# Reciprocal sums of an attention tile turned narrow and early, and spread through DRAM

## What is computed

```python
scores = scale * np.matmul(q, k.transpose(0, 1, 3, 2))
scores = np.where(keep, scores, -1000000000.0)
scores = scores - np.max(scores, axis=-1, keepdims=True)
a = np.exp(scores)
a = a / (np.sum(a, axis=-1, keepdims=True) + 1e-09)
return np.matmul(a, v).astype(np.float32)
```

## Time and profile before

| | |
|---|---|
| median of 3 runs | 562.24 us (561.69 to 562.94) |
| the profiled execution, its own time | 562.56 us |
| its span, first to last instruction | 560.8 us |
| granted TensorE clock, mean | 0.997 |
| attention on TensorE (first scores to first product of the next layer) | 6.28 to 85.29 us |
| DMA, mean | 174 GB/s |

### The profile page before, as it was taken

How to read it: one execution, slowest core, us unless ns; L and a number is a source line. 1 busy time by engine, 2 the same in 40 slices (tenths; PEclk the granted TensorE clock), 3 DMA queues, 4 the chain that set the end, 5 groups by cost and what they waited for, 6 DMA issues and landing times.

```text
span 560.8 us, 10736 instructions
## 1 busy us (share of the span) xinstructions
PE 545.4 (97%) x3830; PEld 454.4 (81%) x3830; DVE 237.2 (42%) x665; ACT 178.1 (32%) x421; POOL 102.5 (18%) x161
## 2 busy tenths in 40 slices
PE   7999999999999999999999999999999999999993
PEld 5776777888888888888888888888788888888882
DVE  5777771333323333332432353733651451454141
ACT  5777762121202212121233334422410330343030
POOL 6234457111100111100000010010211111111111
PEclk9999999999999999999999999999999999999998
DMA  8997522566678766645053111771155597396101
GB/s 231 273 286 215 163 92 79 160 221 202 212 221 249 220 203 219 201 156 161 0 217 121 56 57 59 272 286 57 68 204 191 191 343 300 128 335 223 41 29 28
DMA packets 41637, 97.71 MB, mean 174 GB/s; under 512 B 2864, under 2 KB 15152, under 8 KB 37504
## 3 DMA queue, kind: packets, MB, share of 16 engines
q1 hardware_dynamic: 24912, 61.24, 31.8%
q10 hardware_dynamic: 14128, 27.90, 17.2%
q0 software_dynamic: 2560, 8.09, 4.3%
HBM read 61.11 MB, written 36.10 MB: 173 GB/s over the span
## 4 chain that ended last, share of the span: by engine, by line
PE 96%; DVE 1%; issue 1%; ACT 1%; POOL 0%; DVEq 0%; POOLq 0%
PE bank L1516 14%; PE bank L1311 12%; PE bank L1313 12%; PE bank L1315 12%; PE bank L1388 6%; PE bank L1392 6%; PE bank L1390 6%; PE bank L1297 4%; PE bank L1530 4%; PE bank L1528 4%; PE bank L1529 4%; PE bank L1274 3%; PE bank L1253 3%; PE bank L1408 2%; PE bank L1267 1%
## 5 line engine op out<-in xcount | busy, mean ns | idle before, releaser
L1311 PE MATMUL bank<-x_hi,w_hi 128*128 128x512 f32 x288 | 112.2, 390 | 0.6 <-issue 0.6
L1315 PE MATMUL bank<-x_hi,w_lo 128*128 128x512 f32 x288 | 112.1, 389 | 0.0
L1313 PE MATMUL bank<-x_lo,w_hi 128*128 128x512 f32 x288 | 112.0, 389 | 0.0
L1516 PEld LDWEIGHTS bank<-xgT,w_sb 128*128 128x128 f32 x704 | 80.2, 192 | 1.9 <-issue 0.8
L1516 PE MATMUL bank<-xgT,w_sb 128*128 128x96 f32 x704 | 80.2, 275 | 0.7 <-ACT xgT L856 0.7
L1030 DVE TENSOR_TENSOR sig<-sig,bank 128x512 f32<-128x512 f32 x36 | 24.8, 688 | 128.2 <-ACT sig L751 128.2
L751 ACT ACTIVATE sig<-bank 128x512 f32<-128x512 f32 x36 | 21.5, 598 | 156.9 <-PE bank L1315 156.9
L1311 PEld LDWEIGHTS bank<-x_hi,w_hi 128*128 128x128 f32 x288 | 54.1, 188 | 12.1 <-issue 1.0
L1315 PEld LDWEIGHTS bank<-x_hi,w_lo 128*128 128x128 f32 x288 | 54.1, 188 | 11.4
L1313 PEld LDWEIGHTS bank<-x_lo,w_hi 128*128 128x128 f32 x288 | 54.1, 188 | 11.1
L1388 PE MATMUL bank<-wo_hi,hh_hi 128*128 128x512 f32 x132 | 53.6, 406 | 0.0
(11 more groups left out here) (172 smaller groups left out, 748.5 us busy)
## 6 DMA issues: line engine op xcount, KB each, us to landing
expert_rows<-pad ACTq DMA_DIRECT2D x10, 2698.5 KB, 15.8
w_raw<-w SPq DMA_DIRECT2D x16, 1024.0 KB, 6.7
w_sb<-w SPq DMA_DIRECT2D x16, 1024.0 KB, 7.6
w_raw<-w_gv SPq DMA_DIRECT2D x12, 512.0 KB, 10.7
va_sb<-v_long SPq DMA_DIRECT2D x10, 512.0 KB, 3.9
vb_sb<-v_tail SPq DMA_DIRECT2D x10, 320.0 KB, 5.7
k_sb<-kT SPq DMA_DIRECT2D x12, 256.0 KB, 6.3
wo_raw<-w_out SPq DMA_DIRECT2D x12, 256.0 KB, 11.5
```

The lines of the kernel that those rows point to most:

```text
L1311: nc.tensor.matmul(ps[:, :], w_hi[:, u, a, k, :], x_hi[:, k, tok], start=(k == 0), stop=False)
L1313: nc.tensor.matmul(ps[:, :], w_hi[:, u, a, k, :], x_lo[:, k, tok], start=False, stop=False)
L1315: last = nc.tensor.matmul(ps[:, :], w_lo[:, u, a, k, :], x_hi[:, k, tok], start=False, stop=(k == KD - 1))
L1516: last = nc.tensor.matmul(ps, w1_sb[u][:, k, fc], xgT[:, k * ET:k * ET + ET], start=(k == 0), stop=(k == KD - 1))
```

## The change

Three things are changed. The reciprocals `rsum` are transposed as they are, 128 x 8 in one piece, and ScalarE copies 8 x 128 to `rsumT`. GpSimd's queue writes that to a DRAM tensor `sum_rows`, waits for the landing, and reads it back twice, each time spread over 64 partitions, into one of two `rbc_sb` buffers; VectorE's Q writes the even heads ahead of the odd ones, so that each read is one contiguous row of 512. And the order is another: Q stands at the end of the group behind that of the tile's last scores, R in the next group ahead of its T steps, X one group later than before. `rsum_wide` and its copy on GpSimd are gone. GpSimd's copy of the sinks and its splits keep their places relative to the tiles, behind the new transfers.

```diff
--- before.py
+++ after.py
@@ -66,25 +66,25 @@
         for n in (g, g + 1):
             if n < PAIRS:
                 steps.append(("S", n // HP, n % HP, n))
-        for n in (g - 7, g - 6):
+        for n in (g - 9, g - 8):
             if 0 <= n < PAIRS and n % HP == HP - 1:
                 steps.append(("X", n // HP, None, n // HP))
+        if g >= HP and (g - 3) % HP == HP - 1 and g - 3 < PAIRS:
+            steps.append(("R", (g - 3) // HP, None, psum_use))
+            psum_use += 1
         for n in (g - 3, g - 2):
             if 0 <= n < PAIRS:
                 steps.append(("T", n // HP, n % HP, psum_use))
                 turned[psum_use] = n
                 psum_use += 1
-                if n % HP == HP - 1:
-                    steps.append(("Q", n // HP, None, n // HP))
         for n in (g - 5, g - 4):
             if 0 <= n < PAIRS:
                 tile, hp = divmod(n, HP)
                 steps.append(("V", tile, hp, None))
-                if hp == HP - 1:
-                    steps.append(("R", tile, None, psum_use))
-                    psum_use += 1
                 if tile in EARLY and hp == 1:
                     steps.append(("W", tile, None, tile - EARLY[0]))
+        if 0 < g <= PAIRS and (g - 1) % HP == HP - 1:
+            steps.append(("Q", (g - 1) // HP, None, (g - 1) // HP))
     v_use = itertools.count()
     return [(k, t, h, next(v_use)) if k == "V" else (k, t, h, n) for k, t, h, n in steps], turned
 
@@ -112,6 +112,7 @@
             return ctx.enter_context(nc.semaphore(name))
 
         expert_rows = nc.dram_tensor("expert_rows", (FILLS * FILL, ROW), F32).ap()
+        sum_rows = nc.dram_tensor("sum_rows", (NT, H, P), F32).ap()
 
 
         base = -(-nc.sbuf_base // 64) * 64
@@ -130,8 +131,8 @@
         scores_sb = place("scores_sb", (P, 4, SC), 0, 50.75)
         probsT = place("probsT", (P, TURNED, 4 * P), 0, 54.5)
         xT = place("xT", (P, 2, DM), 2, 0)
-        rbc_sb = place("rbc_sb", (P, DM), 2, 4)
-        rsum_wide = place("rsum_wide", (P, DM), 2, 6)
+        rbc_sb = place("rbc_sb", (P, 2, DM), 2, 4)
+        rsumT = place("rsumT", (P, 2, P), 2, 17)
         h_sb = place("h_sb", (P, NT, FT1, P), 0, 0)
 
 
@@ -276,7 +277,8 @@
         probs_ready = sem("probs_ready")
         pT_in_psum = sem("pT_in_psum")
         pT_by_act, pT_by_dve = sem("pT_by_act"), sem("pT_by_dve")
-        rsum_ready, rsum_spread = sem("rsum_ready"), sem("rsum_spread")
+        rsum_ready, rsum_out = sem("rsum_ready"), sem("rsum_out")
+        rbc_in = [sem("rbc_in0"), sem("rbc_in1")]
         pv_done = sem("pv_done")
         sums_step = sem("sums_step")
         silu_step = sem("silu_step")
@@ -601,17 +603,28 @@
             make_mask(1)
             make_mask(0)
             find_wide()
-            for tile in range(NT):
-                if tile == QT - 1:
+            def spread_sums(tile):
+                use = next(n for kind, t, _, n in ORDER if kind == "R" and t == tile)
+                pool.wait_ge(pT_by_act, evacuated(use)[1])
+                pool.dma_start(sum_rows[tile, :, :], rsumT[0:H, tile % 2, :]).then_inc(rsum_out, 16)
+                pool.wait_ge(rsum_out, tile * 16 + 16)
+                if tile >= 2:
+
+                    pool.wait_ge(o_ready, tile - 1)
+                for u in range(2):
+                    pool.dma_start(rbc_sb[u * D:u * D + D, tile % 2, :],
+                                   sum_rows[tile, u * HP:u * HP + HP, :].rearrange("h q -> (h q)").unsqueeze(0)
+                                   .broadcast_to([D, DM])).then_inc(rbc_in[tile % 2], 16)
+
+            for tile in range(NT + 1):
+                if tile < NT:
+                    spread_sums(tile)
+                if tile == QT - 2:
                     copy_sinks(1)
-                pool.wait_ge(rsum_ready, tile + 1)
-                nc.gpsimd.tensor_copy(rsum_wide.rearrange("p (h c) -> p h c", h=H),
-                                      rsum[:, tile % 2, :].unsqueeze(2).broadcast_to([P, H, D])).then_inc(rsum_spread, 1)
                 if tile:
                     split_x(tile - 1)
-                    if tile - 1 in EARLY:
-                        split_w(tile - 1 - EARLY[0])
-            split_x(NT - 1)
+                if tile - 1 in EARLY:
+                    split_w(tile - 1 - EARLY[0])
 
             with pool.Fori(0, FT1 // 2) as j:
                 for u in range(2):
@@ -718,9 +731,11 @@
                                          ).then_inc(pT_by_act, 1)
                 elif kind == "R":
                     a.wait_ge(pT_in_psum, n + 1)
-                    if tile:
-                        a.wait_ge(o_ready, tile)
-                    nc.scalar.activation(rbc_sb, pT_ps[n % 2][:, :], ACT.Copy).then_inc(pT_by_act, 1)
+                    if tile >= 2:
+
+                        a.wait_ge(rsum_out, (tile - 1) * 16)
+                    nc.scalar.activation(rsumT[0:H, tile % 2, :], pT_ps[n % 2][0:H, 0:P], ACT.Copy
+                                         ).then_inc(pT_by_act, 1)
                 elif kind == "W":
                     split_half(n // 2, n % 2, 16)
 
@@ -950,18 +965,18 @@
                                           ).then_inc(pT_by_dve, 1)
                 elif kind == "Q":
                     d.wait_ge(probs_ready, tile * H + H)
-                    nc.vector.tensor_scalar(rsum[:, tile % 2, :], sums[:, qt % 2, :], 1e-9, None, ALU.add
+                    nc.vector.tensor_scalar(rsum[:, tile % 2, :].rearrange("p (u h) -> p h u", u=2),
+                                            sums[:, qt % 2, :].rearrange("p (h u) -> p h u", u=2), 1e-9, None, ALU.add
                                             ).then_inc(sums_step, 1)
                     d.wait_ge(sums_step, tile + 1)
                     nc.vector.reciprocal(rsum[:, tile % 2, :], rsum[:, tile % 2, :]).then_inc(rsum_ready, 1)
                 elif kind == "X":
-                    use = next(m for k, t, _, m in ORDER if k == "R" and t == tile)
                     d.wait_ge(pv_done, LAST_V[tile] + 1)
-                    d.wait_ge(pT_by_act, evacuated(use)[1])
+                    d.wait_ge(rbc_in[tile % 2], tile // 2 * 32 + 32)
                     if tile >= 2:
 
                         d.wait_ge(xT_ready, tile - 1)
-                    nc.vector.tensor_tensor(xT[:, tile % 2, :], o_ps[tile % 2][:, :], rbc_sb, ALU.mult
+                    nc.vector.tensor_tensor(xT[:, tile % 2, :], o_ps[tile % 2][:, :], rbc_sb[:, tile % 2, :], ALU.mult
                                             ).then_inc(o_ready, 1)
 
             with if_wide(d):
@@ -1262,10 +1277,8 @@
                         by_act, count = evacuated(n - 2)
                         pe.wait_ge(pT_by_act if by_act else pT_by_dve, count)
                     if kind == "R":
-                        pe.wait_ge(rsum_spread, tile + 1)
-                        for hp in range(HP):
-                            last = nc.tensor.transpose(pT_ps[n % 2][:, hp * P:hp * P + P],
-                                                       rsum_wide[:, hp * P:hp * P + P], ident[:, :])
+                        pe.wait_ge(rsum_ready, tile + 1)
+                        last = nc.tensor.transpose(pT_ps[n % 2][0:H, 0:P], rsum[:, tile % 2, :], ident[:, :])
                     else:
                         pe.wait_ge(probs_ready, tile * H + h * 2 + 2)
                         for u in range(2):
```

## The result

The changed kernel takes 592.61 us (median of 4 runs, 590.08 to 594.99) against 562.59 for the kernel before in the same comparison: ratio 1.0534, 95% interval 1.048 to 1.0587. That is 30 us slower, more than twice the 13.3 that were forecast, and outside the range. The profiled execution took 594.07 us with a span of 592.1, 31.3 above the span of before.

What follows compares the result with a forecast made beforehand. TensorE, busy 97% of the span, was taken to bound the kernel. A tile of 8.14 us against 6.72, ten loops, less 0.7 saved, gave +13.5, rounded to 13.3: 562.24 + 13.3 = 575.5 us, range 570 to 584.

Steps and rivals of the forecast that it cites:

- the stall: In the attention, TensorE's second T step waits for ScalarE's R copy behind four exponentials: 1.67 us a tile, plus 0.42.
- The sum: Whole kernel: median 562.24 plus 13.3 gives 575.5 us; ends of this case 571.5 to 579.3.
- That costs 0.1, beside the same chain, so nothing: A tile's first V waits for X, now of its own group: X ends about 2.5, TensorE comes at 2.42.
- the forecast's chain: Attention loop through VectorE, ScalarE's exponentials, R's copy, T and two V steps: 8.14 us a tile against 6.72.
- X until Q at 33.25 (0.60), Q until the T copy at 33.56 (0.31): VectorE times read from the second group's timeline before the change: X takes 0.60 us, Q 0.31, counted in the new order.
- VectorE's term of 4.01 us: From a group's scores' start until VectorE can begin the stalled group's maxima: 0.63 + 1.19 + 0.60 + 1.28 + 0.31.
- The clock: Rival, chance 0.03: TensorE busy 75% in the attention, a third of tiles at 12 us, +16 on the forecast, 591.
- The transfers: GpSimd's DRAM write and reads at 2.7 us each: 6.1 us from R's copy to filled buffer, hidden within 11.1.
- The end: Last tile's sums before the next product's third chunk: about 7 or 9 us, covered by 11.7.
- late transfer: Rival, chance 0.17: X waits for DMAs landing in 6.2 us, 583 us, or 590 and more if reads are slow themselves.
- The no-stall rival: Chance 0.06: no T-step wait in the attention, only the removed transposes count, 8.0 us faster, 554.2 us.

Runs made afterwards that it cites:

- R first, no transfers: Changed kernel with R ahead of its group's scores, Q behind the previous group's scores, X multiplying by ones: attention ends at 84.4 us, against 85.3 in the kernel before.
- Q early: Changed kernel with only Q moved, right behind its group's scores and ahead of X, transfers kept: 586.0 us, ratio 1.0407 to the kernel before.
- X early and no transfers: Changed kernel with R ahead of its group's scores, Q behind the scores, X one group earlier, ones for sums: attention ends at 81.3 us, tiles 6.14 and 6.86.
- stall-alone run: Changed kernel with Q right behind its group's scores and X multiplying by ones, nothing sent through DRAM: attention ends at 101.5 us, late tiles 8.43, clock 1.00.
- run without transfers: Changed kernel, order kept, with X multiplying by ones written once and nothing sent through DRAM: attention ends at 112.0 us, against 113.5 in the changed kernel.

## Why the prediction was wrong

**The direction and the stall were right.** TensorE's T step waits for R's copy in eleven places, as forecast. Taking that wait away (R first, no transfers) takes the whole loss away once the transfers are gone too. Where Q is hardly disturbed and X waits for no transfer, R followed R after 8.14, 8.34 and 8.27 us in the changed kernel (Q's first instruction at 0.16, 0.17 and 0.29); forecast 8.14.

**The sum failed in these terms**, one put behind the other in the order in which the runs take them off:

- The stall alone: 16.2 us, not 13.3; a loop of 8.43, not 8.14. Of the 0.29, 0.08 is the T step, which behind a wait takes 0.58 or 0.59, not 0.51. The other 0.21 belongs to that run's own order: "That costs 0.1, beside the same chain, so nothing", of the first V's wait for X, measured 0.4 with Q ahead of X, and then on the chain. The changed kernel has X ahead of Q, so for it the forecast's chain was sized nearly right.
- **"X until Q at 33.25 (0.60), Q until the T copy at 33.56 (0.31)" was carried over to Q's new place.** This is the step that failed most. In the kernel before Q ran while GpSimd was idle; behind the two T copies it runs beside `x_lo`, and waits for it: 0.95 in place of 0.16. VectorE's term of 4.01 us thus measured 4.71. The forecast listed what VectorE executes in the group, but not what GpSimd executes at that moment. Q's place costs 10.5 us (112.0 - 101.5). As an estimate, half of it is the longer loop, 8.92 against 8.43 ten times, and half the clock, five low stretches at the 1.05 us worked out below.
- The clock was a rival with a chance of 0.03; it came on top. In the runs without transfers it fell in five stretches with Q late, and in none with Q early. Whole executions agree: their mean clock was 0.987 to 0.988 in four of Q early and 0.973 to 0.981 in four of the changed kernel. With Q late a tile took 9.97 or 9.98 with a low stretch and 8.92 without, so a stretch costs about 1.05 us; the forecast had priced 4 a tile. Its argument, that 79% busy had gone with a clock of 1.00, was read from the first 14 us; later stretches, here and without transfers, with 9.5 to 11.7 us busy in 14 went with either clock, and a low clock itself makes the busy time longer.
- The transfers: 1.5 us on top in the changed kernel, though the 2.7 us taken for each was too short. The writes took 1.6 to 6.4 us, 3.5 in the median, and the reads 4.3. X did wait for them, in the early tiles. It cost little because the stalls had made every tile two microseconds longer and so gave the transfers time. Four pairs of runs bear this out: where a late tile without transfers takes 8.92, 8.43, 6.75 and (with X a group earlier) 6.14 us, adding them costs 1.5, 4.6, 14.2 and 27.3 us in the attention, what the clock loses included.
- The end: "hidden" was right for the third chunk (it starts 12.2 us after the first, 11.9 before), but GpSimd's drain wasn't looked at: 2.9.

With 0.3 for the gap between the first two chunks, 16.2 + 10.5 + 1.5 + 0.3 + 2.9 = 31.4, against 31.3 measured in the spans. The parts depend on the order in which they are taken off.

**The form failed too.** The rivals were priced as alternatives, each with a chance, but stall and late transfer don't exclude each other, and either idles TensorE, after which its clock fell. In this kernel all three came, and the range held only the first with a part of the second.

**The no-stall rival** priced the gain at 0.67 a tile; 0.59 was there to be had with X early and no transfers. No path through DRAM that was tried delivers the sums in time for it.

The rule of the Trainium skill that was weighed, that transposes don't count as busy for the clock ("TensorE: Matmul & The Clock Gate", Part 4: PE-mode transpose), is not borne out. The clock did fall in the changed kernel, but filling the stall with transposes alone kept it at 1.00 in all tiles but the early ones.

**Open.** Why the clock held in the stall-alone run at much the same busy share at which it fell elsewhere isn't settled; each of those is one trace. In the run without transfers the loops of 8.92 have the same two waits of TensorE, 0.75 for Q and 1.56 for R's copy, and the clock fell in some of them and not in others. The 8.92 loops and Q's end with `x_lo` show that VectorE's small instruction waited for GpSimd's, not by what means.

## What to carry to other kernels

When a step is moved in an order that several engines walk, look for each wait in its new place at everything that stands ahead of the releaser on its own engine: a copy of 0.25 us behind four exponentials of the same group is a wait of 1.6. Price a moved instruction by what the other engines run beside it at the new moment, and add the losses up instead of choosing among them, since a longer loop hides transfers and a TensorE that waits more can lose its clock as well. Before sending work around TensorE, try the cheap reorder: moving R behind both V steps gave 2.2 us with nothing else changed.

## What was not expected of the hardware

A VectorE instruction from SBUF to SBUF on 128x8 took up to 1.07 us beside GpSimd's 128x512 subtraction and 0.16 to 0.17 away from it. In the run without transfers all nine that started beside such a subtraction ended 0.03 us after it. It is not so for each VectorE instruction: the reciprocal on the same 128x8, next in line, took 0.20 us beside it and away from it, and the copies out of PSUM (0.68) and the mask with its maximum (0.37) kept their times too. GpSimd's final drain grows with the number of DMAs that its queue has issued: 3.10 us before, 4.08 with 12 more, 6.04 with 36 more, 0.08 us each. A write of 4 KB to DRAM on GpSimd's queue took 1.6 us when little else was under way and up to 7.6 when the loads filled the queues.
